# The last GEMM of a fused attention and MLP kernel: transposed result, half of K by Strassen's products; and a narrower stationary operand for the weighing

## What is computed

```
scores = cap * tanh(scale * q @ k.T / cap)
x = softmax(scores) @ v                       # laid out as 896 tokens x 768
h = x @ w_in; x = max(0.01 * h, h) @ w_out    # 768 -> 2048 -> 768
xn = x / sqrt(mean(x * x) + 1e-6) * rms_g
g, val = xn @ w_gate, xn @ w_val              # 768 -> 1536 each
out = (silu(g) * val) @ w_out2                # 1536 -> 768, the last GEMM
```

## Time and profile before

| | |
|---|---|
| median of three runs | 576.0 us |
| profiled execution | 574.06 us |
| its span (first to last instruction) | 572.3 us |
| PE busy | 567.6 us, 99% |
| DVE busy | 357.0 us, 62% |
| ACT busy | 277.6 us, 49% |
| POOL busy | 271.9 us, 48% |
| granted clock of TensorE | 1.00 of full |

### The profile page before, as it was taken

The page is one execution under the profiler, slowest core; times in us unless marked ns, Lnnn a source line. Parts: engine busy times, 40 slices in busy tenths (PEclk is TensorE's granted clock), DMA queues, the critical chain, the costliest instruction groups (busy, mean ns, idle before and its releaser), DMA issues.

```text
span 572.3 us, 7765 instructions
## 1 busy us (share of the span) xinstructions
PE 567.6 (99%) x2823; PEld 493.5 (86%) x2823; DVE 357.0 (62%) x484; ACT 277.6 (49%) x453; POOL 271.9 (48%) x236
## 2 busy tenths in 40 slices
PE   8999999999999999999999999999999999999998
PEld 5555655799999999999999999999999999999997
DVE  4479897685555455326974699988788878511120
ACT  6889888236544454437533555333445435311110
POOL 1036373569665633226643487755688855000000
PEclk9999999999999999999999999999999999999999
DMA  6355432213112222120210011611111114000001
GB/s 170 95 173 164 116 102 65 43 49 111 57 55 67 98 85 57 55 56 27 84 55 29 2 55 57 218 58 56 57 56 55 56 60 162 29 27 29 29 27 56
DMA packets 30006, 41.49 MB, mean 73 GB/s; under 512 B 17040, under 2 KB 18832, under 8 KB 29968
## 3 DMA queue, kind: packets, MB, share of 16 engines
q1 hardware_dynamic: 29824, 40.99, 22.9%
q10 hardware_dynamic: 144, 0.00, 0.0%
HBM read 38.15 MB, written 2.80 MB: 72 GB/s over the span
## 4 chain that ended last, share of the span: by engine, by line
PE 98%; DMA 1%; DVE 1%; issue 0%; DVEq 0%
PE ps L1358 45%; PE ps L1425 21%; PE ps L1516 15%; PE ps L1295 10%; PE ps L1283 4%; PE ps L1301 2%; PE ps L1287 2%; DMA qk_raw<-in_qk 1%; PE ps L1477 0%; PE ps L1500 0%; DVE qk_lo L986 0%; DVE qk_lo L991 0%; DVE r_bc L1262 0%; DVE qk_hi L984 0%; DVE capc L999 0%
## 5 line engine op out<-in xcount | busy, mean ns | idle before, releaser
L518 POOL TENSOR_TENSOR w_lo<-w_raw,w_hi 128x384 fp32r<-128x384 f32 x92 | 107.2, 1169 | 133.8 <-ACT w_hi L632 133.5
L1358 PE MATMUL ps<-x_hi,w_hi 128*128 128x448 f32 x420 | 154.2, 367 | 0.0
L1358 PE MATMUL ps<-x_hi,w_lo 128*128 128x448 f32 x420 | 153.4, 365 | 0.0
L1358 PE MATMUL ps<-x_lo,w_hi 128*128 128x448 f32 x420 | 153.4, 365 | 0.0
L518 POOL TENSOR_TENSOR w_lo<-s_sum,w_hi 128x384 fp32r<-128x384 f32 x80 | 89.1, 1121 | 45.1 <-ACT w_hi L632 44.9
L1358 PEld LDWEIGHTS ps<-x_hi,w_hi 128*128 128x128 f32 x420 | 78.9, 188 | 7.6 <-issue 1.1
L1358 PEld LDWEIGHTS ps<-x_hi,w_lo 128*128 128x128 f32 x420 | 78.9, 188 | 6.3
L1358 PEld LDWEIGHTS ps<-x_lo,w_hi 128*128 128x128 f32 x420 | 78.9, 188 | 6.1
L632 ACT ACTIVATE w_hi<-s_sum 128x384 fp32r<-128x384 f32 x80 | 41.6, 523 | 76.9 <-PE ps L1358 67.9
L1295 PE MATMUL ps<-probs,v_ones 128*128 128x448 f32 x144 | 56.8, 542 | 0.0
L632 ACT ACTIVATE w_hi<-w_raw 128x384 fp32r<-128x384 f32 x92 | 47.3, 515 | 7.5 <-PE ps L1358 7.0
(11 more groups left out here) (145 smaller groups left out, 915.8 us busy)
## 6 DMA issues: line engine op xcount, KB each, us to landing
w_raw<-in_w_out SPq DMA_DIRECT2D x24, 384.0 KB, 3.1
w_raw<-in_w_in SPq DMA_DIRECT2D x16, 384.0 KB, 3.6
qk_raw<-in_qk SPq DMA_DIRECT2D x11, 480.0 KB, 4.2
w_raw<-in_w_gate SPq DMA_DIRECT2D x12, 384.0 KB, 3.0
w_raw<-in_w_val SPq DMA_DIRECT2D x12, 384.0 KB, 3.7
v_ones<-in_v SPq DMA_DIRECT2D x12, 224.0 KB, 3.3
recip_row<-recips SPq DMA_DIRECT2D x12, 224.0 KB, 3.4
v_raw<-in_w_out SPq DMA_DIRECT2D x4, 384.0 KB, 6.4
```

The costliest lines, as they stand in the source:

```text
L518: pool.tensor_tensor(w_lo[:, c], source, w_hi[:, c].bitcast(F32), ALU.subtract).then_inc(w_lo_done, 1)
L1358: last = pe.matmul(ps[:, base(s) + BANK_OF[j], 0:S], w[:, w_c], x[:, xs(j, c)], start=(j in (P1, P5, P7, P6) and c == 0 and w is w_hi and ...
```

## The change

The last GEMM gives its result turned: features on partitions, tokens (two batches of 448) in the free dimension, and the host's view of the output is transposed. Stationary is now w_out2, moving the act_full tiles. It runs in three units of 15 pieces of nine 128x448 matmuls: for the first six tiles of K four plain block products in two halves each (PA, PB, PC, PD with two batches each: eight pieces), for the other six Strassen's seven products. The inverse root is now a row `r_bc`, multiplied by DVE. The seven blocks of x for the Strassen half (T1 to T4 formed by DVE in place in act_full, upper parts by ACT, lower parts by DVE) are made during the last gate and value unit (`UNITS - 1`) and the first unit of the last GEMM (`UNITS`); the parts of the plain half two at a time in the six units before. The weighing's stationary slice is `D + 1` = 65 columns wide.

```diff
+    LAST = UNITS + KH
+    LAST_ORDER = [PA, P1, P5, PB, P7, PC, P6, PD, P3, P2, P4]
+    F0 = N2 // 2
...
# sync: raw weights, four loads for each unit; stores of a unit behind the loads of the next
+            def load_last(s):
+                m, r = s - UNITS, raw_of(s) - 1
+                for k, (row, half) in enumerate(((m, 0), (m, 1), (m + KH, 1), (m + KH, 0))):
+                    load_raw(r + k, w_out2[row, half])
...
# gpsimd
             for s in range(U1 + 2, UNITS):
                 for j in range(7):
                     weight_lo(widx(s, j))
-                    if U1 + 7 <= s < U1 + 7 + EARLY and j in (P5, P3):
-                        value_lo_half(s - U1 - 7, int(j == P3))
-            for k in v2_pool[EARLY:]:
-                value_lo(k)
+                    if s >= UNITS - F0 and j in (P5, P3):
+                        plain_lower_half(2 * (s - UNITS + F0) + int(j == P3))
+            for n in range(W_LAST, len(count)):
+                weight_lo(n)
...
# scalar
+            s = UNITS
+            keep_p1(s - 1)
+            last_weights(s, PA)
+            z_upper(B11)
+            last_weights(s, P1)
+            z_upper(T1)
+            last_weights(s, P5, PB, P7)
+            silu(s - 1, 1)
+            last_weights(s, PC)
+            z_hi(T2, 0)
+            z_hi(T2, 1)
+            silu(s - 1, 0)
+            z_hi(T3, 0)
+            z_hi(T3, 1)
+            z_hi(T2, 2)
+            z_hi(T3, 2)
+            last_weights(s, P6)
+            keep_p1(s)
+            z_upper(B22)
+            z_upper(B21)
+            last_weights(s, PD, P3, P2, P4)
+            z_upper(T4)
...
# vector, the last gate and value unit and the first unit of the last GEMM
+            s = UNITS - 1
+            take_p5(s)
+            for c in range(KH):
+                z_lo(B11, c)
+            take_p7(s)
+            s_part(s + 1, P5)
+            take_p6(s)
+            s_part(s + 1, P7)
+            value_22(s)
+            z_lo(T1, 0)
+            z_lo(T1, 1)
+            gate_sum(s)
+            gate_12(s)
+            z_lo(T1, 2)
+            z_t2(0)
+            z_t2(1)
+            weighted_1(s)
+            gate_11(s)
+            z_t2(2)
+            value_21(s)
+            for c in range(KH):
+                z_t3(c)
+            weighted_0(s)
+            s_part(s + 1, P6)
+            s_part(s + 1, P3)
+            for c in range(KH):
+                z_lo(T3, c)
+
+            s = UNITS
+            take_p5(s)
+            for c in range(KH):
+                z_lo(T2, c)
+            take_p7(s)
+            for c in range(KH):
+                z_t4(c)
+            for c in range(KH):
+                z_lo(B22, c)
+            take_p6(s)
...
+            def result_21(s):
+                dve.wait_ge(prod_done, count[widx(s, P4)])
+                dve.tensor_tensor(u2[s % 2][:, :], bank(s, BANK_D), u2[s % 2][:, :], ALU.add).then_inc(c21_done, 1)
+                dve.wait_ge(c21_done, s + 1)
+                dve.tensor_tensor(u2[s % 2][:, :], u2[s % 2][:, :], r_bc[:, cols(0)], ALU.mult).then_inc(o_done, 1)
...
# tensor
-                    pe.matmul(ps[:, pv_bank(p) + h, 0:S], v_ones[p % 2][:, c:c + 128],
+                    pe.matmul(ps[0:D + 1, pv_bank(p) + h, 0:S], v_ones[p % 2][:, c:c + D + 1],
...
+            def plain(s, row, b, half):
+                j = ((PA, PB), (PC, PD))[row][half]
...
+                    elif (row, b) == (0, 1):
+                        pe.wait_ge(a_done, s + 1)
+                    elif (row, b) == (1, 0):
+                        pe.wait_ge(a2_done, s + 1)
+                    else:
+                        pe.wait_ge(u2_done, s + 1)
...
+            for s in range(UNITS, LAST):
+                plain(s, 0, 0, 0)
+                product(s, P1)
+                product(s, P5)
+                plain(s, 0, 0, 1)
+                plain(s, 0, 1, 0)
+                product(s, P7)
+                plain(s, 0, 1, 1)
+                plain(s, 1, 0, 0)
+                product(s, P6)
+                plain(s, 1, 0, 1)
+                plain(s, 1, 1, 0)
+                plain(s, 1, 1, 1)
+                for j in (P3, P2, P4):
+                    product(s, j)
```

More of the change, by code:

```diff
@@ L129, in build @@
         SPARE = place["at"]
[L131 to L147, removed]
+        at(G)
+        act_lo = buf("act_lo", N2 * B * S, F32R)
+        at(RING)
+        plain_ring = buf("plain_ring", 8 * S, F32R)
+        at(SPARE)
+        plain_spare = buf("plain_spare", 4 * S, F32R)
         ps = ctx.enter_context(nc.psum_tensor("ps", [128, 8, 512], F32))
@@ L364, in pieces_of @@
[L364 to L380, removed]
+        PLAIN = [(k, b) for b in range(B) for k in range(F0)]
@@ new lines, in build, with act_tile, plain_hi, plain_lo @@
+        plain_count = {part: i + 1 for i, part in enumerate(PLAIN)}
+        def act_tile(k, b):
+            return act_full[:, cols(2 * k + b)]
+        def plain_hi(k, b):
+            i = PLAIN.index((k, b))
+            return plain_ring[:, cols(i)] if i < 8 else plain_spare[:, cols(i - 8)]
+        def plain_lo(k, b):
+            return act_lo[:, cols(2 * k + b)]
+        def z_tile(blk, c):
+            return {B11: act_tile(F0 + c, 0), T3: act_tile(F0 + c, 0), B21: act_tile(F0 + KH + c, 0),
+                    B22: act_tile(F0 + KH + c, 1)}.get(blk, act_tile(F0 + c, 1))
@@ L482, in _, with store @@
                 load_raw(raw_of(U1 + f) + 1, w_val[f])
[L483 to L503, removed]
+            def load_last(s):
+                m, r = s - UNITS, raw_of(s) - 1
+                for k, (row, half) in enumerate(((m, 0), (m, 1), (m + KH, 1), (m + KH, 0))):
+                    load_raw(r + k, w_out2[row, half])
+            def store(s):
+                for kind in range(4):
+                    row, b, tile = result(s, kind)
+                    row = s - UNITS + KH * row
+                    sp.wait_ge(o_done, 4 * (s - UNITS) + kind + 1)
+                    sp.dma_start(out[row * 128:(row + 1) * 128, cols(b)], tile[:, :]).then_inc(out_sem[kind], 16)
+            load_last(UNITS)
+            load_last(UNITS + 1)
+            store(UNITS)
+            load_last(UNITS + 2)
+            store(UNITS + 1)
+            store(UNITS + 2)
+            for kind in range(4):
+                sp.wait_ge(out_sem[kind], 16 * KH)
         @block.gpsimd
@@ new lines, in _ @@
+            for c in range(KH):
+                z_t3(c)
+            weighted_0(s)
+            s_part(s + 1, P6)
+            s_part(s + 1, P3)
+            for c in range(KH):
[7 more added lines that the diff above has]
+                z_t4(c)
+            for c in range(KH):
+                z_lo(B22, c)
+            take_p6(s)
+            for blk in (B21, T4):
+                for c in range(KH):
+                    z_lo(blk, c)
@@ L1264, in _ @@
+            result_22(s)
+            s_parts(s + 1)
+            result_12(s)
+            result_11(s)
+            result_21(s)
+            for s in range(UNITS + 1, LAST):
+                take_p5(s)
+                take_p7(s)
+                take_p6(s)
+                result_22(s)
+                if s + 1 < LAST:
+                    s_parts(s + 1)
+                result_12(s)
+                result_11(s)
+                result_21(s)
         @block.tensor
```

313 lines of the change are left out of this document (162 added, 151 removed).

## The result

The changed kernel takes 586.17 us in the median of four runs (586.00 to 586.88), the kernel before 576.21 (575.09 to 576.74): a ratio of 1.0178, interval 1.016 to 1.0196. I had forecast 573.7 and a range of 570.3 to 577.0.

A forecast was written before the change was run, and what follows sets the result against it. PE was taken as the bound from end to end. -6.0 (matmuls) + 3.2 (wait for take_p5) + 1.05 (end) - 0.6 (weighing) = -2.35 us on 576.0 gave 573.7 us, range 570.3 to 577.0.

The forecast's parts named there:

- Matmuls: Last GEMM: 405 matmuls instead of 504, at 0.2027 us each, so 6.0 us less.
- What else is moved, and what hides it: ScalarE, GpSimd, VectorE and raw-weight work around the last GEMM: claimed hidden, adding nothing to the sum.
- Raw weights: Loads behind the last gate weights and one unit later: claimed to leave as before, at no cost.
- my 3.2 us: PE's wait before the first last-GEMM unit's fifth piece, from four GpSimd hits on VectorE; bounds 0 and 4.8 us.
- The wait for take_p5: First unit of the last GEMM, fifth piece: PE waits for VectorE's full queue, 3.2 us, bounds 0 and 4.8.
- take_p6: First unit's eleventh piece: six VectorE instructions before this bank read cause no wait, with cover of 0 to 0.8 us.
- The clock: Rival, chance 0.14: PE's clock halves in the wait before the fifth piece, 1.82 us per piece; 577.3 us with two.
- The end: Behind the last matmul: 3.8 us to the span's end, 1.05 us more than before; bounds 0.8 and 1.4.
- The weighing: Attention weighing: a 65-column load shortens one exposed load in each of 12 pairs, 0.6 us less in all.

The follow-up runs named there:

- e2: The changed kernel with ScalarE making the upper parts of the plain half one unit earlier; 576.09 us, ratio 1.0021 to the kernel before.
- e5: e2 with six VectorE instructions moved behind the first unit's take_p5, and ScalarE keeping P1 before weight P6's upper part; 575.61 us, ratio 0.9996.
- e4: e1 with VectorE making take_p5 of the first unit before the three lower parts of T3; 576.51 us, ratio 1.0018.
- e3_weighing_only: The kernel before with only the weighing's stationary operand narrowed to 65 columns; 574.9 us, ratio 0.9994.
- e9: e5 with keep_p1 directly behind the last silu on ScalarE and take_p6 before the lower parts of B22 on VectorE; 571.18 us, ratio 0.9924.
- e8: The changed kernel with the VectorE and ScalarE order of e5, but upper parts of the plain half left late; 584.5 us, ratio 1.0151.
- e1: The changed kernel with GpSimd making the plain half's two lower parts behind all seven weights of a unit; 578.7 us, ratio 1.0055.

## Why the prediction was wrong

**Matmuls.** 405, as counted. Their pace was a little under: the three units end at 526.19, 553.75 and 581.30 us in the changed kernel, 27.55 us for 135, or 0.2041 us each instead of 0.2027. The plain pieces are the slower ones (5.54 us for 27, the Strassen ones 5.48). 0.6 us less gain than forecast, inside the bounds.

**The step that failed** is in "What else is moved, and what hides it": "nine instructions, about 11 us in a unit of 12.77. A weight's place is free 11 us before its next use, which covers that." I counted GpSimd's work and did not ask what each of its instructions waits for. plain_lower_half of a pair waits for plain_upper, which ScalarE makes behind the last weight of the unit; GpSimd wants it behind the second weight. So GpSimd stood still for 2 us in each of six units and then had both lower parts and seven weights to make in a row, the cover of 11 us was gone, and PE lost 4.4 us where the sum had nothing. The prediction should have laid the two queues side by side: the instruction's place in one and its releaser's place in the other. The sentence behind it, "Raw weights: two loads behind the last gate weights and two one unit later, as before", failed by the same cause: the loads wait for a weight's lower part and left at 483.96 instead of about 471 (the expectations say 486). That made VectorE idle for 4.48 us, and GpSimd's late weights stood beside VectorE's three lower parts of B11, which took 4.11 us instead of 2.52 in e2. Together this turned my 3.2 us into 7.7. e2 undoes this one wait and nothing else, and gives back 9 of the 10 us lost. Its trace is 11.0 us shorter than the changed kernel's: 4.4 by the six gaps, 4.0 by the wait before the fifth piece, 1.2 by the one in the third, 0.7 by the clock, and 0.7 that its first gate and value unit starts sooner, which is not of this cause.

**The wait for take_p5.** Place and cause were right (released by L972, VectorE's queue full ahead of it, no wait at P7). The size was right once the other fault was gone: 3.7 us in e2, inside 0 to 4.8. From take_p5 to take_p5 VectorE took 19.3 us there (473.19 to 492.48) against 15.5 without hits: 3.8 of lengthening, where four hits had been given 3.2.

**take_p6.** "So no wait, but the cover is thin": in e5 its six instructions on SBUF took 7.2 us, and PE waited 1.9 us. In the changed kernel the earlier wait hid it.

**The clock.** I gave 0.14 to its fall. It fell to the lower of its two levels, 1.2 GHz, in every trace with a gap of 3.9 us or more and cost 1.4 to 2.7 us, seven to fifteen matmuls at 0.373 instead of 0.203. I had priced it at 1.82 for each piece of nine; at 0.17 a matmul it is 1.5, and 0.8 to 1.7 pieces were hit. The rule of the Trainium skill's page "TensorE: Matmul & The Clock Gate", section "HAM oscillation — how this bites in real kernels", that short gaps of PE are harmless and longer ones lower the clock, agrees with these traces: 2.0 us harmless, 3.9 not. The clocks of all executions draw no such sharp line: with the gap of 3.9 us in the trace, one of e2's ten and two of e4's ten executions show 1.000, and in e5, whose longest gap in the trace is 2.3 us, six of twelve show a fall.

**The end.** 3.8 us behind the last matmul's end, as forecast (581.30 to 585.1), against 2.76 before. The last matmul and the last product with r_bc:

```profile
580.94 0.36 PE L1473 MATMUL ps<-x_hi,w_lo 128*128 128x448 f32 x1
...
582.00 0.62 DVE L1270 TENSOR_TENSOR u<-u,r_bc 128x448 f32<-128x448 f32 x1
```

**The weighing.** 0.05 us in each pair, 0.4 in sum in the trace of e3_weighing_only, 0.6 forecast; in the run times not to be told from nothing. The record of the load of L1301 takes 132 ns there instead of 184.

**What was right in the whole.** With the one wait mended, e2 lies inside the range but not on the gaining side: 0.8 us over the kernel before beside it, where 2.35 less had been forecast. Its profiled span is 1.8 us longer than before (574.1 against 572.3), which leaves 4.15 us to explain: 1.5 are the clock, 0.5 the longer wait, 0.6 the pace, and 1.45 come from the second GEMM of the MLP, which starts 0.85 us later (208.62 against 207.77) and not 0.6 sooner. The cause of that last term is open. With the reads first (e9) the last GEMM gains, and the whole change is worth 4.5 us, 0.8%.

## What to carry to other kernels

When work is put into a queue between two instructions that others need, look up where in its own queue its releaser stands; GpSimd, with 11.6 us of work in a unit of 12.8, was hidden in e2, where no upper part made it wait, and not in the changed kernel, where it stood for 1.9. On an engine that both empties banks and prepares operands, put each bank read at the place where the bank is filled, and the preparation behind it: the same instructions in other orders had ratios of 1.0021, 0.9953, 0.9996 and 0.9924 to the kernel before. A wait of PE has a second price, the clock behind it: one wait of 3.7 us cost 1.5 us more in e2. In the trace of e5 three waits of 4.0 us in sum cost no clock, but half of its executions show that it fell, so splitting a wait is no sure way round.

## What the runs showed of the hardware

VectorE's instructions that read two tensors from SBUF and GpSimd's hold each other up: beside GpSimd's weights three of VectorE's took 4.03 us (L1235 in e5) where three take 1.68 with GpSimd idle (L1230 in e9), and of GpSimd's four weights there the three behind the first took 1.38 to 1.40 us, the first 1.01. VectorE's that read PSUM took 0.61 to 0.62 in all these rows.

The clock falls neither at once nor after a fixed wait. Behind PE's last matmul before the gap it went to half after 2.0 us in the changed kernel (at 498.1), 2.6 in e4, 3.8 in e8 and 4.9 in e1. In e2 it fell after 4.6 us, when PE had been back for 1.1: five matmuls behind the gap started at the full pace and nine more at half of it. The changed kernel by stretches of 1 us, columns as in e9's row above (the clock is the third from the end; PE stands still):

```profile
497.00:498.00 1.00, 0.00 (x0) 0.00 (x0) 1.00 (x3) 0.07 (x1) 0.00 (x0) 1.00 0.00 0
498.00:499.00 1.00, 0.00 (x0) 0.00 (x0) 1.00 (x3) 1.00 (x3) 0.00 (x0) 0.53 0.00 0
499.00:500.00 1.00, 0.00 (x0) 0.00 (x0) 0.92 (x2) 0.98 (x3) 0.00 (x0) 0.50 0.00 0
```
